# Tap products of a local-attention kernel: the multiplication walks channel outside and tap inside, and the softmax weights are stored tap inside

## What is computed

```python
# x (4, 4160, 192), weight_gen (4, 4160, 8, 7)
w = exp(weight_gen - max over the 7 taps);  w = w / (sum over the 7 taps + 1e-9)
x_pad = 6 rows of zeros in front of each sequence
out[b, s, h, g] = sum over k of w[b, s, h, k] * x_pad[b, s + k, h, g]     # 8 heads x 24 channels
# expert: w_in (192, 1024), conv_w (3, 1024), w_out (1024, 192)
h = maximum(out @ w_in, 0)
conv_out[s] = conv_w[0] * h[s - 1] + conv_w[1] * h[s] + conv_w[2] * h[s + 1]
result = (h * sigmoid(conv_out)) @ w_out
```

## Time and profile before

| | us |
|---|---|
| median of 3 runs | 788.49 (787.89 to 789.17) |
| the profiled execution | 786.22 |
| its span | 784.4 |
| PE busy in it | 701.6 (89%) |
| DVE busy | 675.3 (86%) |
| POOL busy | 611.4 (78%) |
| ACT busy | 523.9 (67%) |
| the 138 products of POOL (L280) | 380.7, mean 2.768 |
| the 119 gating products of POOL (L417) | 197.9, mean 1.663 |

### The profile page before, as it was taken

How to read it: one execution, slowest core, us unless ns; L and a number is a source line. 1 busy time by engine, 2 the same in 40 slices (tenths; PEclk the granted TensorE clock), 3 DMA queues, 4 the chain that set the end, 5 groups by cost and what they waited for, 6 DMA issues and landing times.

```text
span 784.4 us, 12158 instructions
## 1 busy us (share of the span) xinstructions
PE 701.6 (89%) x4008; PEld 672.9 (86%) x4008; DVE 675.3 (86%) x648; ACT 523.9 (67%) x719; POOL 611.4 (78%) x308
## 2 busy tenths in 40 slices
PE   0116698999999999989999899999999998999998
PEld 0016598999999999989999899999999998999998
DVE  3898999898999898998989998989989898985650
ACT  1117678676687676786667876678767678676761
POOL 1889999888888888998879888889878888852320
PEclk9999799999999999999999999999999999999999
DMA  7820130303323031303124030313123030000001
GB/s 155 173 54 1 30 78 16 83 21 82 78 51 72 20 82 38 91 15 83 48 50 107 21 77 20 82 41 82 42 55 79 24 90 18 20 16 21 18 26 36
DMA packets 31292, 43.11 MB, mean 55 GB/s; under 512 B 8551, under 2 KB 28614, under 8 KB 28872
## 3 DMA queue, kind: packets, MB, share of 16 engines
q1 hardware_dynamic: 31270, 42.82, 22.0%
HBM read 30.03 MB, written 12.78 MB: 55 GB/s over the span
## 4 chain that ended last, share of the span: by engine, by line
PE 81%; DVE 8%; ACT 4%; issue 3%; DMA 2%; POOL 1%; SPq 0%; ACTq 0%; DVEq 0%; POOLq 0%
PE out_ps L700 42%; PE z L686 34%; DVE attn L588 3%; PE turn_ps L711 3%; DMA x_win<-in_x 2%; PE z L742 2%; DVE z L558 1%; POOL weighted L280 1%; ACT hidden L460 1%; ACT L478 1%; ACT gated L478 1%; DVE z L564 1%; DVE weighted L280 1%; ACT xa_hi L496 0%; DVE wb_lo L547 0%
## 5 line engine op out<-in xcount | busy, mean ns | idle before, releaser
L280 POOL TENSOR_TENSOR weighted<-x_win,soft 120x1344 f32<-120x1344 f32 x138 | 380.7, 2768 | 55.4 <-DVE attn L588 44.2
L700 PE MATMUL out_ps<-wo,gated 128*128 128x192 f32 x2016 | 352.4, 328 | 8.1 <-ACT out_sb L503 8.1
L700 PEld LDWEIGHTS out_ps<-wo,gated 128*128 128x128 f32 x2016 | 327.6, 187 | 22.7 <-ACT out_sb L503 15.4
L417 POOL TENSOR_TENSOR gated<-gated,hidden 128x832 f32<-128x832 f32 x119 | 197.9, 1663 | 87.4 <-ACT gated L478 87.4
L588 DVE TENSOR_REDUCE attn<-weighted 120x192 f32<-120x1344 f32 x140 | 215.9, 1545 | 5.3 <-POOL weighted L280 3.3
L460 ACT ACTIVATE hidden<-z 128x836 f32<-128x836 f32 x160 | 138.7, 867 | 100.7 <-PE z L686 92.0
L558 DVE SCALAR_TENSOR_TENSOR z<-hidden,cw,z 128x832 f32<-128x832 f32 x160 | 173.1, 1082 | 16.4 <-ACT z L467 15.2
L564 DVE SCALAR_TENSOR_TENSOR z<-hidden,cw,z 128x832 f32<-128x832 f32 x160 | 174.0, 1088 | 4.3
L467 ACT ACTIVATE z<-hidden,cw 128x832 f32<-128x832 f32 x160 | 153.4, 959 | 5.2
L686 PE MATMUL z<-xa_hi,wa_hi 128*128 128x418 f32 x320 | 103.5, 405 | 20.8 <-ACT gated L478 9.3
L478 ACT ACTIVATE gated<-z 128x832 f32<-128x832 f32 x119 | 102.4, 861 | 27.0 <-DVE z L564 25.8
(11 more groups left out here) (43 smaller groups left out, 378.2 us busy)
## 6 DMA issues: line engine op xcount, KB each, us to landing
x_win<-in_x SPq DMA_DIRECT2D x18, 1170.0 KB, 7.9
out<-out_sb SPq DMA_DIRECT2D x127, 96.0 KB, 1.6
logits<-in_weight_gen SPq DMA_DIRECT2D x18, 183.8 KB, 9.0
x_win<-in_x SPq DMA_DIRECT2D x2, 1160.2 KB
wo<-in_moe_w_out SPq DMA_DIRECT2D x1, 768.0 KB, 15.9
gated<-in_moe_w_in SPq DMA_DIRECT2D x1, 512.0 KB, 5.6
gated<-in_moe_w_in SPq DMA_DIRECT2D x2, 256.0 KB, 16.4
mask<-in_masks SPq DMA_DIRECT2D x20, 23.0 KB, 1.7
```

Source lines behind the costliest of these rows:

```text
L280: return engine.tensor_tensor(y, rows, s, ALU.mult)
L417: nc.gpsimd.tensor_tensor(to, to, hidden[:, (c.ring * J + j) % RING, 1:1 + CHUNK], ALU.mult) \
L700: last = nc.tensor.matmul(out_ps[0:end - u * P, 0:D], gated[:, j, u * P:end], wo[:, j, :], start=(j == 0), stop=(j == J - 1))
```

## The change

Three places change, all in the way in which operands are walked. `soft` is stored head outside and tap inside (i h k) by L266, and L272 follows. `multiply` walks head, channel, tap, with the tap inside: the write to `weighted` takes its elements in the order in which they lie, the weights are read along their 7 taps and again for each of the 24 channels, and x is read at steps of one row, 192 elements, for 7 taps, then again from the next channel. Buffers, sizes, values, engines and waits stay.

```diff
@@ normalise
-            engine.tensor_tensor(soft[0:PA, :].rearrange("p (i k h) -> p i h k", i=GROUP, k=K), e, r,
+            engine.tensor_tensor(soft[0:PA, :].rearrange("p (i h k) -> p i h k", i=GROUP, k=K), e, r,
                                  ALU.mult).then_inc(s_norm, 1)
...
-            s = soft[0:PA, :].rearrange("p (a h) -> p a h", h=H)
-            m = mask[0:PA, c.ring, :].unsqueeze(2).to_broadcast([PA, GROUP * K, H])
+            s = soft[0:PA, :].rearrange("p (i h k) -> p i h k", i=GROUP, k=K)
+            m = mask[0:PA, c.ring, :].rearrange("p (i k) -> p i k", k=K).unsqueeze(2).to_broadcast([PA, GROUP, H, K])
@@ multiply
-            s = soft[0:PA, i * K * H:(i + 1) * K * H].rearrange("p (k h) -> p k h", h=H).unsqueeze(3) \
-                .to_broadcast([PA, K, H, G])
-            rows = x_win[0:PA, c.ring, i * D:(i + K) * D].rearrange("p (k h g) -> p k h g", k=K, h=H)
-            y = weighted[0:PA, (c.ring * GROUP + i) % RING, :].rearrange("p (h g k) -> p k h g", h=H, k=K)
+            s = soft[0:PA, i * K * H:(i + 1) * K * H].rearrange("p (h k) -> p h k", h=H).unsqueeze(2) \
+                .to_broadcast([PA, H, G, K])
+            rows = x_win[0:PA, c.ring, i * D:(i + K) * D].rearrange("p (k h g) -> p h g k", k=K, h=H)
+            y = weighted[0:PA, (c.ring * GROUP + i) % RING, :].rearrange("p (h g k) -> p h g k", h=H, k=K)
```

## The result

| | before | after |
|---|---|---|
| median of the runs, us | 788.19 (4 runs) | 884.69 (4 runs, 883.58 to 886.26) |
| profiled execution, us | 786.22 | 886.26 |
| its span, us | 784.4 | 884.5 |
| mean granted clock of TensorE | 0.993 | 0.959 |

The changed kernel takes 1.123 times as long, 95% interval 1.1208 to 1.1252: 96.5 us more. The forecast was 838, the range 784 to 880. The direction was right; the loss is 96.5 us where 50 was forecast, and the time lies 4.7 us above the range.

What follows compares the result with a forecast made beforehand. PE was taken to bound the kernel before, POOL after the change. POOL's start 18.7, own work 593.0, waits 3, end 81 and 138 x 1.00 us gave a span of 833.7; plus 4.1, 838 us, range 784 to 880.

Steps and rivals of the forecast that it cites:

- The bound and the slack: Steady turn of 106.23 us: PE bounds, POOL has 12.6 us of slack, so each of 21 products may grow 0.60 us.
- POOL's waits: POOL's waits of 44.2 us for DVE and 35.7 for ACT nearly vanish once POOL is the bound; 3 us left.
- Rival C: Product takes 3.60 us but POOL's waits stay: 926 us, its sign turns over 120 us; chance 0.06.
- The price of the product: Each of 138 products on POOL takes 3.60 us from start to start, 1.00 us more than now.
- the likeliest case: POOL's product at 3.48 to 3.75 us makes POOL the bound: 818 to 862 us, chance 0.55.
- The sum: Whole run: 18.7 + 593.0 + 3 + 81 + 138 x 1.00 = 833.7 us span, plus 4.1 gives 838.
- the case of 3.75 us: On POOL, x's stepped read takes 1.79 ns and the weight 0.84 after it: product 3.75 us, time 859 us.
- The end: After POOL's last product the sum follows at once: 1.5 + 79.4 = 81 us to the end.
- The softmax weights: On POOL, normalising loses its write step, at most 1 us back; mask product keeps adjacent elements; nothing counted.
- DVE's products in the fill: Two products on DVE, 2.56 and 4.05 us, move their step to a read: 1 us less or more each, nothing taken.
- Rival A: POOL's read step is hidden, product 2.48 to 2.60 us: 785 to 789 us; under 3.20 only some us in the fill; chance 0.22.
- Rival B: The 768-byte step costs more or short weight runs pay too: POOL's product over 3.9 to 5.03 us, up to 1035; chance 0.17.

Runs made afterwards that it cites:

- experiment 2: Changed kernel with the new walk only in POOL's products of three of seven tokens, the old walk in the others: 797.34 us, ratio 1.0140 to before.
- experiment 3: Changed kernel with the new walk only in POOL's products of four of seven tokens, the old walk in the others: 817.67 us, ratio 1.0395 to before.
- experiment 4: Changed kernel with each head's first-tap weight used for all 7 taps, so the weight rests while x stays stepped: 798.88 us, ratio 1.0161 to before.
- experiment 9: Changed kernel with one gating product in eight moved from POOL to DVE: 855.71 us, ratio 1.0863 to before.
- experiment 6: Changed kernel with POOL's products in all pairs of x and weight walks, rate only: 2.50 us (in order, one weight), 3.99 (changed walk), 2.71 (walk of before).
- experiment 10: Changed kernel with two moving operands in most of POOL's products, rate only: stepped x beside x in order 3.75 us, both stepped at the same addresses 2.61.
- experiment 1: Changed kernel with the old walk back in POOL's products, softmax weights stored as changed: 787.70 us, ratio 1.0008 to before.
- experiment 12: Changed kernel with POOL's products reading x twice in equal walks at different addresses, rate only: stepped 3.39 to 5.02 us, in order 1152 elements apart 3.08.
- experiment 5: Changed kernel with POOL's products reading x at steps of 1 to 192 elements beside one weight, rate only: 2.50 us at step 2, 3.55 at 24, 3.19 at 192.

## Why the prediction was right and wrong

- **The bound and the slack: right.** PE with 12.6 us of slack for POOL per turn, and a switch at 0.60 us per product. Experiments 2, 3 and 4, with +0.57, +0.76 and +0.47 us in the mean, give turns of 107.05, 109.76 and 106.98 us: 0.8 us over before on the near side of the switch, 3.5 beyond it. Experiment 9 shows the bound from the other side.
- **POOL's waits vanish, so that its own work counts: right.** They went from 79.9 to 4.0 us, and POOL is busy 99% of a turn. Rival C is out, although its sign, a turn over 120 us, came about: with waits that stay, 27.9 us for 21 products of 1.33 make a turn of 134.1 us, without them 121.5, and 120.38 was measured.
- **The price of the product: the term that failed.** The prediction said 3.60 us from start to start, +1.00; it is 3.93, +1.33, and 1.30 over the whole run. In the likeliest case it put the whole price on the step of x (DVE's 0.74 ns per element for the low value, a single access of 1.79 ns for the high one) and nothing on the weights' new walk beyond an unstepped read. The runs put this in its place: the step of x beside a resting weight costs 0.70 us over a product without any step (3.20 for 2.50), less than was taken, and the weights' walk, taken at nothing, costs 0.79 us beside it (3.99 for 3.20; 0.80 in experiment 4). Less the 0.21 that the write's step had cost this is 1.28, the 3.99 less 2.71 of experiment 6. The split depends on the order of counting: by experiment 10, with x in order as the second operand, the step makes 1.25 us and the weights' runs another 0.24. What of the 0.79 is the runs and what the second operand's moving at all stays open.
- **The sum: part of it is luck.** The median of 884.69 lies 47 us over 838. The product makes 41 of them, the end 8, POOL's waits and its later start 1.5; the median lies only 0.2 us above the profiled span where 4.1 were added, which takes 4 back. In the same way the case of 3.75 us, at 859, misses by 26 us: 20 for the product, 8 for the end, 1.5 for waits and start, less the same 4. The prediction's sum with +1.33 gives 883.3 us, but its nearness is a cancelling of these, not a sum without errors.
- **The end: 8 us too short.** The last 79.4 us were right to the tenth: PE turns the last sums at 805.06 and ends at 884.5. But the sum doesn't follow the last product at once. DVE takes it in its own step, 6.9 us after the product's end, since by the program POOL's products run two steps (AHEAD) ahead of the steps in which DVE sums them.
- **The softmax weights: the sign of one half was not foreseen.** L266 lost 45 ns as said, L272 gained 106, and its mask is now read in runs of 7 where it rested before: probably the same effect, in an instruction that I had counted as unchanged. Experiment 1 shows both hidden.
- **DVE's products in the fill: right**, 2.44 us for 2.56 at the first, 2.90 for 4.05 at the second, which is 1.15 less where 1 was the bound. (For DVE's write step of 8 the prediction's 0.28/392 is 0.71 ns, not 0.73; nothing hangs on it.)
- **Rival A: wrong in its price.** "Some us in the fill at most" was 9.2 us in the fill of experiment 4 at +0.47 us per product, and 12 us in all. The fill has little slack, and that stands in the earlier trace rows: POOL busy 70.86 of 80 us.
- **Rival B** came about by its own words: a product over 3.9 us, 3.93 measured. Of its reasons it was the second, that the weights' reading pays too; the length of the step is not borne out. Its upper bound of 5.03 us, both reads paying, was reached in experiment 12 (4.98, 5.02) by two stepped reads.
- **PE's busy time** was forecast to stay at 104 us a turn; it is 108.79, at a granted clock of 0.97 where it was 1.00. It is not what sets the turn, since POOL is busy 119.58 of its 120.38 us.

"GPSIMD Engine Reference", section "Performance pitfalls for Q7 kernels", of the Trainium skill gives one cycle more per element for a step over 8 bytes. The place of the limit agrees with experiment 5 (8 bytes free, 12 bytes not). The size, an estimate of 1.12 us by that page, holds for one of the steps only: beside a resting operand it was 0.40 us at 12 bytes, 1.05 at 96 and 0.70 at the 768 of the changed kernel. The measurement decides.

## What to carry to other kernels

When a transposing walk has to put its step somewhere, put it where the same instruction is already slow for another reason: here it costs 0.21 us in POOL's write, 0.70 in its read beside a resting weight and 1.49 with the weights' new walk, and 1.01 in DVE's sum. Cost both operands of a two-input instruction together: a change that makes a resting operand move can cost as much as the step itself, 0.79 us here. And read slack by stage: a turn forgave 0.60 us per product, the fill next to nothing.

## What the runs showed of the hardware that was not expected

- On POOL a stepped read's price depends on where the other operand reads: step 192 took 2.61 us with both operands at the same addresses, 3.20 with one element, 3.75 with an operand in order, 4.98 with another stepped one 4 elements on. Why two operands in order 1152 elements apart took 3.08 us, where they took 2.43 (median) at the same addresses, stays open; the distance was not varied there. That both move does not explain it: the gating product reads two tiles in order and took 1.66 us for 832 elements, 1.6 ns per element by an estimate with some 0.3 us fixed, as the 2.43 us give (1.6) and not as the 3.08 (2.1).
- The price rises with the step from 12 bytes to 96 (2.90, 3.11, 3.27, 3.55 us for steps of 3, 4, 8 and 24 elements) and is lower again at 768 bytes in runs of 7 (3.19). Run length and step were not varied apart, so which of the two lowers it stays open.
- A subtraction of DVE with two SBUF inputs waited for POOL's products. In the timeline of DVE in the fill of the changed kernel, the same subtraction alone (first row) and beside POOL's longer products:

```profile
5.63 0.57 DVE L259 TENSOR_TENSOR logits<-logits,top 120x392 f32<-120x392 f32 x1
...
52.05 2.86 DVE L259 TENSOR_TENSOR logits<-logits,top 120x392 f32<-120x392 f32 x1
...
55.41 3.65 DVE L259 TENSOR_TENSOR logits<-logits,top 120x392 f32<-120x392 f32 x1
```

It took 0.57 us alone and 2.86 and 3.65 us beside products of 4 us; in the kernel before, whose products are shorter, the worst was 1.47. "SBUF — State Buffer", section "Who interferes with whom", of the Trainium skill says that such an instruction contends with a POOL instruction that reads SBUF, and that the shared ports are an exclusive lock; the trace agrees: POOL's product from 54.44 ends at 58.64, and the DVE subtraction of 55.41 ends at 59.06, some 0.4 us behind it.
